# Reordering the work at the phase ends of an expert-choice mixture kernel

## The chip, the cores and the metric

The kernel runs on one core of one Trainium2 chip. The metric is the device time of one execution in microseconds (us), the median of the runs. Engines are named as in the profile: PE (TensorE matmuls), PEld (its weight loads), DVE (VectorE), ACT (ScalarE), POOL (GpSimd) and SP (SyncE, which only issues DMAs here).

## The reference

Three layers follow each other. An attention with gates and a running state gives 3072 token rows of 320 values. A mixture of 8 experts follows, each of which takes exactly 384 tokens: the pairs (token, expert) are taken in the order of their logit, and a pair is passed over if the token has an expert or the expert is full. The last layer multiplies two projections of each row and projects the product back.

```
logits = x @ w_gate                     # x: 3072 x 320, w_gate: 320 x 8
for idx in argsort(-logits.flatten()):  # greedy, capacity 384 per expert
    ... assigned[token] = expert
for e in range(8):
    h = maximum(x[mask_e] @ w1[e], 0)   # 320 x 1024
    out[mask_e] = h @ w2[e]             # 1024 x 320
a = out @ w_a; b = out @ w_b            # 320 x 1536 each
y = (a * b) @ w_out                     # 1536 x 320
```

## The kernel before

`attention` runs first (to about 200 us of the span) and is not touched. `experts` runs the rest as eight phases, one for each expert in the order in which the experts become full. A phase handles that expert's 384 tokens through both layers, and beside its matmuls the other engines find and fetch the tokens and weights of the next expert.

Every 32-bit operand is held as two parts, a high part (rounded to the matmul's type) and a low part (the rest). A product is summed from high by high, low by high and high by low. ACT writes high parts by a copy, DVE writes low parts by a subtraction that needs the high part first.

A phase k has two loops.

- Eight steps `f` (FT = 8): `up(k, f)` on PE, 8 matmuls into `psA[f % 2]`; ACT's relu writes `h_hi` (L1061); DVE's `h_low` writes `h_lo` (L1320); `down(k, f)` on PE, 9 matmuls into the three accumulators `acc`. PE issues `up(f + 1)` ahead of `down(f)`. `down(k, 0)` waits for `h_lo` and, accumulator by accumulator, for the three output copies of the phase before (`o_copied`, L895).
- Twelve steps `g` (GT = 12): `pair(k, g)` on PE, 16 matmuls into `psA` and `psB`; ACT copies `psA` to `a_sb` (L1080); DVE multiplies into `ab` (L1327); ACT writes `ab_hi` (L1075, `ab_high`); DVE writes `ab_lo` (L1331); `project(k, g)` on PE, 9 matmuls. The two DVE operations are one function, `product(g)`. In its step g, PE issues `pair(g + 1)` and then `project(g)`, DVE does `product(g + 1)`, and ACT does the `a_sb` copy and `ab_high(g)`.

The next expert's work is written into the twelve steps by hand. All engines take their instructions in the written order.

- Step 6: DVE's `rows` writes the row numbers `idx_g`. POOL then issues three gathers of 128 rows each into `xg` (L840), one semaphore each.
- The weights of the next expert come in four quarters q through two raw buffers, quarter q in buffer q % 2, four DMAs on SP each (L818 to L821). SP issues quarter q when the low parts of quarter q - 2 are done. ACT's `high_parts(k + 1, q)` (three copies, L1041 to L1043) waits for the four DMAs; DVE's `low_parts(k + 1, q)` (four subtractions, L1261 to L1268) waits for ACT. The table `SPLIT_AT` says after which step's product each quarter is split, on both engines: quarters 0 and 1 in steps 6 and 7, 2 in step 9, 3 in step 10.
- `widen(k + 1)` on DVE copies 64 columns inside each gathered tile (three copies, L1279), each after its gather has landed. It stands at the start of step 8.
- PE's `turn_tile(k + 1, t)` (L864) transposes gathered tile t into `psT`: tile 0 at the end of step 8, tiles 1 and 2 in steps 9 and 10 between `pair` and `project`. Tile t waits for widening copy t and for the low part of tile t - 1, since all three use `psT`. ACT's `columns(k + 1, t)` (L1033) copies the turned tile to `x1_hi`, DVE's `low(k + 1, t)` (L1284) writes `x1_lo`. DVE does `low(0)` at the start of step 9, `low(1)` and `low(2)` inside `product(10)` and `product(11)`, between its two operations.
- Step 11: PE waits for all of `x1`, issues `up(k + 1, 0)`, then `project(k, 11)`. At the end DVE copies the three accumulators to `o_sb` (L1408) and starts the next phase with `h_low(0)`.
- The search for the expert after next puts more small work on DVE: `leave_out` in step 7 after the product, `propose` in step 8 after it, `propose_rest` in step 9, `keys` in step 11.

The phases 0 to 5 are "search" phases, phase 6 ("rest") has no search, phase 7 prepares nothing. So there are seven phase ends at which a next phase is prepared.

Of the kernel before, what the change touches and what calls it, by code (L numbers as in the profile page):

```python
# [7 lines left out]
ALU = mybir.AluOpType  # L8
# [13 lines left out]
CAP = NT // E  # L22
# [639 lines left out]
ST = TILES // SC  # L662
SPLIT_EARLY = {0: 1, 2: 2, 4: 3}
WO_EARLY = 6
SPLIT_AT = {6: 0, 7: 1, 9: 2, 10: 3}
NG = 6
GJ = TILES // NG
GE = 72
# [2 lines left out]
def experts(nc, ctx, logit, identf, second, w_out, w1, w2, xs, out, fixed):  # L671
# [19 lines left out]
    FT = F1 // P  # L691
# [20 lines left out]
    h_hi = [sb(f"h_hi{n}", [P, CAP], F32R) for n in range(2)]  # L712
    h_lo = [sb(f"h_lo{n}", [P, CAP], F32R) for n in range(2)]
# [315 lines left out]
    @block.scalar  # L1029
    def _(act):  # L1030
        def columns(k, t, ps=psT):
            act.wait_ge(sm["t_done"], T * k + t + 1)
            act.copy(x1_hi[:, :, t * P:(t + 1) * P], ps[:, 0:3 * P].rearrange("p (j n) -> p j n", j=3)  # L1033
                     ).then_inc(sm["x1_hi_ready"], 1)

        def high_parts(k, q):
            n = q % 2
            act.wait_ge(raw_in[n], 64 * (2 * k + q // 2 + 1))
            if not (isinstance(k, int) and k == 0):
                act.wait_ge(sm["x2_mm"], 3 * k)  # L1040
            act.copy(w1_hi[q][:, :, :], w1_raw[n][:, :, :]).then_inc(sm["w_hi_done"], 1)  # L1041
            act.copy(w2_hi[q][:, :, 0:DM], w2_raw[n][:, :, :]).then_inc(sm["w_hi_done"], 1)
            act.copy(w2_hi[q][:, :, DM:], w2_raw[n][:, :, DM - 64:]).then_inc(sm["w_hi_done"], 1)  # L1043

        def high_out(q):
            act.wait_ge(wo_in[q % 2], 16 * (q // 2 + 1))
            act.copy(wo_hi[:, q * GQ:(q + 1) * GQ, :], wo_raw[q % 2]).then_inc(sm["wo_hi_done"], 1)

        high_parts(0, 0)
        for t in range(T):  # L1050
            columns(0, t, acc[t])

        def turn(k, beside):
            early = isinstance(k, int) and k == 0
            for f in range(FT):
                act.wait_ge(sm["up_done"], k * FT + f + 1)

                at_least(act, sm["down_done"], k * (FT - 1) + f - 1)
                if f == 0:
                    at_least(act, sm["x2_mm"], 3 * k)  # L1060
                act.activation(h_hi[f % 2][:, :], psA[f % 2][:, 0:CAP], ACT.Relu).then_inc(sm["h_hi_ready"], 1)  # L1061
                if early and f in SPLIT_EARLY:
                    high_parts(0, SPLIT_EARLY[f])
                if early and f == WO_EARLY:
                    high_out(0)
            for m in range(3):
                act.wait_ge(sm["x2_mm"], 3 * k + m + 1)
                act.copy(x2_hi[:, m, :], acc[m][:, 0:CAP]).then_inc(sm["x2_hi_ready"], 1)

            def ab_high(g):  # L1070
                act.wait_ge(sm["ab_done"], k * GT + g + 1)
                at_least(act, sm["out_done"], k * (GT - 1) + g - 1)
                if g < 2:
                    at_least(act, sm["out_mm"], T * k)
                act.copy(ab_hi[g % 2][:, :], ab[g % 2][:, :]).then_inc(sm["ab_hi_ready"], 1)  # L1075

            for g in range(GT):
                act.wait_ge(sm["ab_mm"], k * GT + g + 1)
                at_least(act, sm["ab_done"], k * GT + g - 1)
                act.copy(a_sb[g % 2][:, :], psA[g % 2][:, 0:CAP]).then_inc(sm["a_copied"], 1)  # L1080

                if beside and g > 9:
                    columns(k + 1, g - 9)
                ab_high(g)
                if early and g < Q - 1:
                    high_out(g + 1)
                if beside and g in SPLIT_AT:
                    high_parts(k + 1, SPLIT_AT[g])
                if beside and g == 9:
                    columns(k + 1, 0)  # L1090
        turns(act, turn)

    @block.vector
    def _(dve):
# [214 lines left out]
        per = ct.n - start + ROUNDS  # L1309
        start -= ROUNDS  # L1310

        def turn(k, beside):

            p = k + 1
            early = isinstance(k, int) and k == 0
            ct.turn(start + p * per)

            def h_low(f):
                dve.wait_ge(sm["h_hi_ready"], k * FT + f + 1)
                dve.scalar_tensor_tensor(out=h_lo[f % 2][:, :], in0=psA[f % 2][:, 0:CAP], scalar=0.0,  # L1320
                                         in1=f32(h_hi[f % 2][:, :]), op0=ALU.max, op1=ALU.subtract).then_inc(sm["h_ready"], 1)

            def product(g, turned=None):

                dve.wait_ge(sm["a_copied"], k * GT + g + 1)
                at_least(dve, sm["ab_ready"], k * GT + g - 1)
                dve.tensor_tensor(ab[g % 2][:, :], a_sb[g % 2][:, :], psB[g % 2][:, 0:CAP], ALU.mult).then_inc(sm["ab_done"], 1)  # L1327
                if turned is not None:
                    low(k + 1, turned)
                dve.wait_ge(sm["ab_hi_ready"], k * GT + g + 1)  # L1330
                dve.tensor_tensor(ab_lo[g % 2][:, :], ab[g % 2][:, :], f32(ab_hi[g % 2][:, :]), ALU.subtract  # L1331
                                  ).then_inc(sm["ab_ready"], 1)

            search = beside == "search"
            h_low(0)
            for f in range(FT - 1):
                if search and f:
                    narrow(p, f - 1)
                if search:
                    tally(p, f)  # L1340
                h_low(f + 1)
                if search:
                    is_full(p, f)
                if early and f in SPLIT_EARLY:
                    low_parts(0, SPLIT_EARLY[f])
                if early and f == WO_EARLY:
                    low_out(0)
            if search:
                narrow(p, FT - 2)
                tally(p, FT - 1)  # L1350
            for m in range(3):
                dve.wait_ge(sm["x2_hi_ready"], 3 * k + m + 1)
                dve.tensor_tensor(x2_lo[:, m, :], acc[m][:, 0:CAP], f32(x2_hi[:, m, :]), ALU.subtract).then_inc(sm["x2_ready"], 1)  # L1353
            if search:
                is_full(p, FT - 1)
                narrow(p, FT - 1)
            product(0)
            for g in range(GT):

                if search and FT + g < ROUNDS:  # L1360
                    tally(p, FT + g)
                    is_full(p, FT + g)
                if beside == "search" and g == 3:
                    give()
                if beside and g in (5, 6):
                    one_hot(p, 0 if g == 5 else SC - 1)
                if beside and g == 8:
                    widen(k + 1)
                if beside and g == 9:
                    low(k + 1, 0)  # L1370
                if g < GT - 1:
                    product(g + 1, g - 8 if beside and g in (9, 10) else None)

                if beside == "search":
                    if FT + g < ROUNDS:
                        narrow(p, FT + g)
                    if g == 3:
                        filled(p)
                    if g == 7:
                        leave_out()  # L1380
                    if g == 8:
                        propose()
                    if g == 9:
                        propose_rest()
                    if g == GT - 1:
                        keys()
                if beside == "rest" and g == 3:
                    the_rest(p)
                if beside and g == 4:
                    places(p)  # L1390
                if beside and g == 5:
                    one_hot(p, 1)
                    one_hot(p, 2)
                if beside and g == 6:
                    rows(p)
                if early and g < Q - 1:
                    low_out(g + 1)
                if beside and g in SPLIT_AT:
                    low_parts(k + 1, SPLIT_AT[g])
            if beside is None:  # L1400

                dve.wait_ge(sm["scattered"], 16 * T * (E - 1))
                dve.tensor_copy(idx_s[:, :], idx_g[:, :]).then_inc(sm["idx_s_ready"], 1)
            for t in range(T):
                dve.wait_ge(sm["out_mm"], T * k + t + 1)

                at_least(dve, sm["scattered"], 16 * T * k)
                dve.tensor_copy(o_sb[:, t, :], acc[t][:, 0:DM]).then_inc(sm["o_copied"], 1)  # L1408
# [39 lines left out]
```

## Time and profile before

| what | value |
|---|---|
| median of 3 runs | 985.36 us (981.37 to 985.89) |
| the profiled execution | 981.72 us |
| its span, first to last instruction | 980.0 us |
| mean granted PE clock | 0.949 of full |
| PE busy | 854.5 us (87%) |
| DVE busy | 650.0 us (66%) |
| ACT busy | 257.3 us (26%) |
| POOL busy | 187.9 us (19%) |

The profile is of one execution. Busy time is a sum of instruction durations; a matmul's end is modelled. In the rows of a timeline, instructions of one engine overlap a little, so that the distance between two starts says more of its pace than a duration does. The bracket at the end of a timeline row is the time that the engine was idle before the row, and who ended it. A "granted clock" of 1.00 is 2.4 GHz, 0.50 is 1.2 GHz.

### The profile page before, as it was taken

To read this page: it belongs to the slowest core of one execution; us is meant where nothing else is said; L and a number is where in the kernel's file an instruction comes from. 1 tells how busy PE (TensorE), PEld (TensorE's weight loads), DVE (VectorE), ACT (ScalarE), POOL (GpSimd) and SP (SyncE) were. 2 spreads that over 40 slices of the span, in tenths; PEclk is the share of its full clock that TensorE was granted. 3 is DMA by queue.
4 is the path that set the end of the run, shared out by engine and by line. 5 is a ranking of instruction groups with operands and counts; after the bars stand their busy time and mean duration, and the time that the engine had idled before them with its cause. 6 is when DMAs were issued, how large, how long until landed. Compare 5 with 4: busy or idle time off the path is not lost.

```text
span 980.0 us, 17872 instructions
## 1 busy us (share of the span) xinstructions
PE 854.5 (87%) x6122; PEld 809.0 (83%) x6122; DVE 650.0 (66%) x1639; ACT 257.3 (26%) x493; POOL 187.9 (19%) x218
## 2 busy tenths in 40 slices
PE   1899999943479979998999899899989998999995
PEld 1899899932378979997898799789978988998995
DVE  7489999975756775577558656855775575265222
ACT  5222222200223331232124123312331242233221
POOL 7466767710100110011001100110110011011001
PEclk9989999965689999999999999999999999999998
DMA  3866667200321220041013001200310040032000
GB/s 88 225 170 186 191 186 212 88 13 11 98 71 41 69 77 14 2 119 41 0 31 107 20 0 59 79 20 0 103 56 0 2 135 21 1 93 67 1 1 21
DMA packets 49722, 66.59 MB, mean 68 GB/s; under 512 B 6592, under 2 KB 43984, under 8 KB 48720
## 3 DMA queue, kind: packets, MB, share of 16 engines
q1 hardware_dynamic: 43856, 54.25, 19.4%
q0 software_dynamic: 2368, 7.88, 2.8%
q10 hardware_dynamic: 3456, 3.93, 1.2%
q8 instruction: 23, 0.38, 0.2%
q14 instruction: 19, 0.16, 0.1%
HBM read 57.88 MB, written 8.16 MB: 67 GB/s over the span
## 4 chain that ended last, share of the span: by engine, by line
PE 46%; DVE 20%; issue 5%; ACT 4%; DMA 1%; POOL 1%; DVEq 0%; ACTq 0%; POOLq 0%
PE psA L875 17%; PE acc L898 11%; PE psB L875 8%; PE acc L923 6%; DVE at_slot L1241 2%; DVE ab L1327 2%; DVE w_lo L1265 2%; ACT ab_hi L1075 2%; DVE w_lo L1261 2%; PE psT L935 2%; DMA xg<-xs_dram,idx_g 1%; DVE w_hi L1263 1%; DVE cmp L1103 1%; PE psT L949 1%; PE psT L943 1%
## 5 line engine op out<-in xcount | busy, mean ns | idle before, releaser
L875 PE MATMUL psA<-x_hi,wa 128*128 128x384 f32 x480 | 135.5, 347 | 0.4 <-DVE x_lo L1353 0.4
L875 PE MATMUL psB<-x_hi,wb 128*128 128x384 f32 x480 | 132.3, 341 | 0.0
L840 POOL DMA_INDIRECT xg<-xs_dram,idx_g x24 | 25.6, 1068 | 499.2 <-DVE idx_g L1255 494.3
L875 PE MATMUL psB<-x_lo,wb 128*128 128x384 f32 x288 | 97.0, 337 | 0.0
L875 PE MATMUL psA<-x_lo,wa 128*128 128x384 f32 x288 | 96.9, 336 | 0.0
L1080 ACT COPY a_sb<-psA 128x384 f32<-128x384 f32 x96 | 46.1, 480 | 188.8 <-PE psB L875 188.7
L923 PE MATMUL acc<-wo_hi,ab_hi 128*128 128x320 f32 x288 | 91.9, 319 | 1.0 <-DVE ab_lo L1331 1.0
L923 PE MATMUL acc<-wo_lo,ab_hi 128*128 128x320 f32 x288 | 88.8, 308 | 0.0
L923 PE MATMUL acc<-wo_hi,ab_lo 128*128 128x320 f32 x288 | 88.7, 308 | 0.0
L1331 DVE TENSOR_TENSOR ab_lo<-ab,ab_hi 128x384 fp32r<-128x384 f32 x96 | 53.5, 558 | 52.3 <-ACT ab_hi L1075 52.1
L1327 DVE TENSOR_TENSOR ab<-a_sb,psB 128x384 f32<-128x384 f32 x96 | 52.9, 551 | 52.4 <-ACT a_sb L1080 52.1
L875 PE MATMUL psA<-x_hi,w_hi 128*128 128x384 f32 x192 | 74.4, 388 | 14.1 <-DVE w_lo L1268 7.5
L875 PEld LDWEIGHTS psB<-x_hi,wb 128*128 128x128 f32 x480 | 86.2, 189 | 0.0
L875 PEld LDWEIGHTS psA<-x_hi,wa 128*128 128x128 f32 x480 | 83.0, 189 | 2.5 <-DVE x_lo L1353 1.1
L1061 ACT ACTIVATE h_hi<-psA 128x384 fp32r<-128x384 f32 x64 | 31.4, 491 | 202.7 <-PE psA L875 202.7
L898 PE MATMUL acc<-h_hi,w_hi 128*128 128x384 f32 x192 | 72.0, 375 | 14.3 <-DVE h_lo L1320 14.3
L1075 ACT CAST ab_hi<-ab 128x384 fp32r<-128x384 f32 x96 | 49.3, 514 | 88.3 <-DVE ab L1327 87.5
L875 PE MATMUL psA<-x_lo,w_hi 128*128 128x384 f32 x192 | 66.4, 346 | 0.0
L898 PE MATMUL acc<-h_hi,w_lo 128*128 128x384 f32 x192 | 66.3, 345 | 0.0
L898 PE MATMUL acc<-h_lo,w_hi 128*128 128x384 f32 x192 | 66.2, 345 | 0.0
L852 POOL DMA_INDIRECT out_dram<-o_sb,idx_s x24 | 23.6, 983 | 220.2 <-DVE o_sb L1408 215.4
L1320 DVE SCALAR_TENSOR_TENSOR h_lo<-psA,h_hi 128x384 fp32r<-128x384 f32 x64 | 34.9, 547 | 30.5 <-ACT h_hi L1061 30.5
(233 smaller groups left out, 1917.3 us busy)
## 6 DMA issues: line engine op xcount, KB each, us to landing
toks<-in_tok_dram SPq DMA_DIRECT2D x24, 484.0 KB, 5.1
w_raw<-in_w_dram SPq DMA_DIRECT2D x32, 320.0 KB, 3.2
w_raw<-in_w_dram SPq DMA_DIRECT2D x32, 256.0 KB, 3.0
qks<-in_qk_dram SPq DMA_DIRECT2D x24, 320.0 KB
w_raw<-in_w_dram SPq DMA_DIRECT2D x64, 64.0 KB, 2.8
xs_dram<-y ACTq DMA_DIRECT2D x24, 160.0 KB, 3.8
qst<-in_qk_dram SPq DMA_DIRECT2D x48, 60.0 KB
piece<-in_w_a_dram SPq DMA_DIRECT2D x6, 256.0 KB, 2.7
```

The lines of the kernel that those rows point to most:

```text
L840: pool.indirect_dma_start(out=xg[:, t, 0:DM], out_offset=None, in_=xrows, in_offset=bass.IndirectOffsetOnAxis(ap=idx_g[:, t:t + 1], axis=0 ...
L852: pool.indirect_dma_start(out=out, out_offset=bass.IndirectOffsetOnAxis(ap=idx_s[:, t:t + 1], axis=0), in_=o_sb[:, t, :], in_offset=None). ...
L875: last = pe.matmul(ps, w, x, start=(n == 0), stop=(n == len(steps) - 1))
L898: last = pe.matmul(acc[m][:, 0:CAP], w[q][:, f % FQ, c], x[n][:, :], start=(f == 0 and j == 0), stop=(f == FT - 1 and j == 2))
L923: last = pe.matmul(acc[t][:, 0:DM], x[n][:, c], w[:, g, :], start=(g == 0 and j == 0), stop=(g == GT - 1 and j == 2))
L935: last = pe.matmul(psG, ohc[:, n * GJ:n * GJ + GE // E, :].rearrange("p j e -> p (j e)"), cmp[:, js, :].rearrange("p j i -> p (j i)"), sta ...
L1061: act.activation(h_hi[f % 2][:, :], psA[f % 2][:, 0:CAP], ACT.Relu).then_inc(sm["h_hi_ready"], 1)
L1075: act.copy(ab_hi[g % 2][:, :], ab[g % 2][:, :]).then_inc(sm["ab_hi_ready"], 1)
L1080: act.copy(a_sb[g % 2][:, :], psA[g % 2][:, 0:CAP]).then_inc(sm["a_copied"], 1)
L1320: dve.scalar_tensor_tensor(out=h_lo[f % 2][:, :], in0=psA[f % 2][:, 0:CAP], scalar=0.0, in1=f32(h_hi[f % 2][:, :]), op0=ALU.max, op1=ALU.s ...
L1327: dve.tensor_tensor(ab[g % 2][:, :], a_sb[g % 2][:, :], psB[g % 2][:, 0:CAP], ALU.mult).then_inc(sm["ab_done"], 1)
L1331: dve.tensor_tensor(ab_lo[g % 2][:, :], ab[g % 2][:, :], f32(ab_hi[g % 2][:, :]), ALU.subtract).then_inc(sm["ab_ready"], 1)
```

## The change

Four edits, all in the order of instructions; no operation is added or left out.

1. Quarter 2 of the weights is split in step 8 instead of step 9, on ACT and on DVE (`SPLIT_AT`).
2. ACT's `columns(k + 1, 0)` moves from the end of step 9 to between its `a_sb` copy and `ab_high(9)`, as tiles 1 and 2 have it.
3. DVE's widening moves from the start of step 8 (before `product(9)`) to the end of step 7, before the low parts of quarter 1.
4. DVE's `h_low(k + 1, 0)` moves in front of the three output copies of phase k.

```
-SPLIT_AT = {6: 0, 7: 1, 9: 2, 10: 3}
+SPLIT_AT = {6: 0, 7: 1, 8: 2, 10: 3}
...
-                if beside and g > 9:
+                if beside and g >= 9:
                     columns(k + 1, g - 9)
                 ab_high(g)
...
                 if beside and g in SPLIT_AT:
                     high_parts(k + 1, SPLIT_AT[g])
-                if beside and g == 9:
-                    columns(k + 1, 0)
...
+        h_low(0, 0)
+
         def turn(k, beside):
...
-            h_low(0)
             for f in range(FT - 1):
...
-                h_low(f + 1)
+                h_low(k, f + 1)
...
-                if beside and g == 8:
-                    widen(k + 1)
                 if beside and g == 9:
                     low(k + 1, 0)
...
+                if beside and g == 7:
+                    widen(k + 1)
                 if beside and g in SPLIT_AT:
                     low_parts(k + 1, SPLIT_AT[g])
+            if beside is not None:
+                h_low(k + 1, 0)
             if beside is None:
```

## Rows read from the trace of the kernel before

**Rows 1.** Waits, whole run: us in total, times, longest us.
```profile
PE acc L898 <- DVE h_lo L1320: 14.3, 7, 2.4
PE psT L864 <- DVE xg L1279: 8.5, 6, 1.6
PE psA L875 <- DVE x_lo L1284: 6.6, 7, 1.2
PE psT L864 <- DVE x_lo L1284: 6.0, 7, 1.7
```

**Rows 2.** Timeline of PE, end of phase 2: start us, us, what.
```profile
530.22 0.55 PE L864 MATMUL psT<-identf,xg 128*128 128x128 f32 x3 [1.51 <-DVE xg L1279]
...
534.13 0.52 PE L864 MATMUL psT<-identf,xg 128*128 128x128 f32 x3 [0.53 <-DVE x_lo L1284]
...
535.80 0.52 PE L875 MATMUL psA<-x_hi,wa 128*128 128x384 f32 x2
...
541.34 0.44 PE L875 MATMUL psA<-x_hi,w_hi 128*128 128x384 f32 x1 [0.89 <-DVE x_lo L1284]
...
548.07 0.44 PE L898 MATMUL acc<-h_hi,w_hi 128*128 128x384 f32 x1 [2.38 <-DVE h_lo L1320]
```

**Rows 3.** Timeline of DVE, the same stretch, from the end of `leave_out`.
```profile
527.23 0.36 DVE L1208 TENSOR_TENSOR tiefree<-tie,free 128x192 f32<-128x192 f32 x1
527.74 0.69 DVE L1261 TENSOR_TENSOR w_lo<-w_raw,w_hi 128x512 fp32r<-128x512 f32 x1
...
529.98 0.39 DVE L1279 COPY xg<-xg 128x64 f32<-128x64 f32 x3
530.29 0.55 DVE L1327 TENSOR_TENSOR ab<-a_sb,psB 128x384 f32<-128x384 f32 x1
...
533.42 0.56 DVE L1284 TENSOR_TENSOR x_lo<-psT,x_hi 128x384 fp32r<-128x384 f32 x1 [0.33 <-ACT x_hi L1033]
...
540.27 0.55 DVE L1327 TENSOR_TENSOR ab<-a_sb,psB 128x384 f32<-128x384 f32 x1
...
544.18 0.17 DVE L1133 TENSOR_SCALAR sign<-best 128x24 int32<-128x24 int32 x1
...
546.18 1.28 DVE L1408 COPY o_sb<-acc 128x320 f32<-128x320 f32 x3
547.38 0.55 DVE L1320 SCALAR_TENSOR_TENSOR h_lo<-psA,h_hi 128x384 fp32r<-128x384 f32 x1
```

**Rows 4.** Timelines of POOL and SP, the same stretch: last gather, last load of quarter 2.
```profile
525.23 0.95 POOL L840 DMA_INDIRECT xg<-xs_dram,idx_g  x1 [0.30 <-issue]
...
526.43 0.44 SPq L821 DMA_DIRECT2D w_raw<-in_w_dram  x1
```

**Rows 5.** Line views: landing of that gather, of that load, of all 24 gathers.
```profile
DMA to landing us min/median/max: 4.3/4.3/4.3
...
DMA to landing us min/median/max: 4.0/4.0/4.0
...
DMA to landing us min/median/max: 3.1/3.7/5.0
```

**Rows 6.** Timeline of ACT, the same stretch.
```profile
531.36 0.83 ACT L1041 CAST w_hi<-w_raw 128x768 fp32r<-128x768 f32 x1
...
532.93 0.46 ACT L1033 CAST x_hi<-psT 128x384 fp32r<-128x384 f32 x1
...
538.83 0.48 ACT L1080 COPY a_sb<-psA 128x384 f32<-128x384 f32 x1 [1.70 <-PE psB L875]
```

**Rows 7.** Timeline of PE at the end of phase 6.
```profile
898.21 0.44 PE L898 MATMUL acc<-h_hi,w_hi 128*128 128x384 f32 x1 [0.21 <-DVE h_lo L1320]
```

**Rows 8.** Windows after phase 1's end: span, engines' busy us, granted clock, DMA, GB/s.
```profile
456.90:457.90 1.00, 1.00 (x10) 0.94 (x11) 0.03 (x1) 0.00 (x0) 0.70 (x2) 0.88 0.15 56
457.90:458.90 1.00, 1.00 (x4) 1.00 (x5) 0.91 (x3) 0.00 (x0) 0.69 (x2) 0.50 0.29 108
...
460.90:461.90 1.00, 1.00 (x7) 0.80 (x6) 0.54 (x3) 0.00 (x0) 0.00 (x0) 0.91 0.00 0
```

More of the change, by code:

```diff
@@ L664 @@
 WO_EARLY = 6
-SPLIT_AT = {6: 0, 7: 1, 9: 2, 10: 3}
+SPLIT_AT = {6: 0, 7: 1, 8: 2, 10: 3}
 NG = 6
@@ L1080, in turn @@
                 act.copy(a_sb[g % 2][:, :], psA[g % 2][:, 0:CAP]).then_inc(sm["a_copied"], 1)
-                if beside and g > 9:
+                if beside and g >= 9:
                     columns(k + 1, g - 9)
@@ L1088, in turn @@
                     high_parts(k + 1, SPLIT_AT[g])
-                if beside and g == 9:
-                    columns(k + 1, 0)
         turns(act, turn)
@@ L1310, in _, with h_low @@
         start -= ROUNDS
+        def h_low(k, f):
+            dve.wait_ge(sm["h_hi_ready"], k * FT + f + 1)
+            dve.scalar_tensor_tensor(out=h_lo[f % 2][:, :], in0=psA[f % 2][:, 0:CAP], scalar=0.0,
+                                     in1=f32(h_hi[f % 2][:, :]), op0=ALU.max, op1=ALU.subtract).then_inc(sm["h_ready"], 1)
+        h_low(0, 0)
         def turn(k, beside):
@@ L1316, in turn @@
             ct.turn(start + p * per)
[L1318 to L1321, printed above, removed]
             def product(g, turned=None):
@@ L1334, in turn @@
             search = beside == "search"
-            h_low(0)
             for f in range(FT - 1):
@@ L1340, in turn @@
                     tally(p, f)
-                h_low(f + 1)
+                h_low(k, f + 1)
                 if search:
@@ L1366, in turn @@
                     one_hot(p, 0 if g == 5 else SC - 1)
-                if beside and g == 8:
-                    widen(k + 1)
                 if beside and g == 9:
@@ L1397, in turn @@
                     low_out(g + 1)
+                if beside and g == 7:
+                    widen(k + 1)
                 if beside and g in SPLIT_AT:
                     low_parts(k + 1, SPLIT_AT[g])
+            if beside is not None:
+                h_low(k + 1, 0)
             if beside is None:
```

## The prediction
> **What bounds the kernel now.** I read the waits of the whole run first. At the seven phase ends TensorE loses time in four places, and these alone name what the change moves: for the next phase's first low part of h (14.3 us), for the widened tile (8.5), for the low part of the last turned tile in front of the next `up` (6.6), and for the low part of the tile before in front of a turning (6.0), together 35.4 us [rows 1]. Then the timelines of one phase end, phase 2's. On TensorE the reader sees the four stalls in their order: 1.51 us before tile 0 is turned, 0.53 before tile 1, 0.89 before `up(k+1, 0)` and 2.38 before `down(k+1, 0)`, 5.3 us in all [rows 2]. On VectorE he sees why: from 527.7 to 547.9 it works nearly without a gap, the longest one shown being 0.33 us [rows 3]. So inside a phase TensorE sets the time, but over the last 20 us of it VectorE does. An order that leaves VectorE more idle there makes the phase longer, whatever it does for TensorE's single waits. Last the transfers, since two edits move a wait for a DMA forward in an in-order queue.
>
> **The widening, one step earlier.** VectorE is done with `leave_out` at 527.6 [rows 3]. The third gather was issued at 525.23 and took 4.3 us, so it lands at 529.5 [rows 4, 5]. Today the widening comes at 529.98 and finds all three landed; in its new place VectorE stands still for 1.9 us with quarter 1's low parts and `product(9)` queued behind. After it the low parts of quarter 1 take 529.98 - 527.74 = 2.24 us: VectorE reaches `product(9)` at 529.7 + 2.2 = 531.9 instead of 530.29. What is gained is that tile 0 can be turned when TensorE comes to it, at 530.22 - 1.51 = 528.7.
>
> **Quarter 2, one step earlier.** ScalarE now comes to quarter 2's high parts before `a_sb(9)`. Quarter 2's last load was issued at 526.43 and took 4.0 us: 530.4 [rows 4, 5]. That issue hangs on the low parts of quarter 0, which stay where they were. ScalarE waits for it, copies for 532.93 - 531.36 = 1.57 us [rows 6] until 532.0, and only then does the `a_sb` copy (0.48): `product(9)` starts at 532.5, 0.6 us behind what VectorE's own queue gives. Cost of this wait alone: 0.6 us; it would be 2 us if the widening weren't late too. Product and `propose` take 533.42 - 0.33 - 530.29 = 2.80 us [rows 3], to 535.3. And now the step that decides: the low parts of quarter 2 (2.24 us) stand in front of `low(0)`, where they used to come behind `product(10)`. `low(0)` starts at 537.6 instead of 533.42. TensorE turns tile 1 0.71 us after that start [rows 2, 3], at 538.3 instead of 534.13, and since `project(9)` and `pair(11)` are queued behind the turning, all of it is 4.2 us late. Edit 2 (`columns(0)` in front of `ab_high(9)`) hides: tile 0 has been turned for 3 us, the copy is over before `ab(9)` is ready. At worst, uncovered, it costs its 0.48 us; at best it gives back the 0.33 us for which `low(0)` waited.
>
> **What is given back.** From tile 1's turning `pair(11)` follows after 1.67 us and `a_sb(11)` 3.03 us later [rows 2, 6]: 543.0, product at 543.5 instead of 540.27 [rows 3], 3.3 us late. VectorE itself is there earlier, at 537.6 + (540.27 - 533.42 - 2.24) = 542.2, so it is TensorE that has it wait. From `ab(11)` to `keys` 3.91 us, `keys` 2.00 us [rows 3]: 549.4. There edit 4 helps. Today three copies (1.20 us) stand before the low part of h and TensorE starts 0.69 us after its start, 1.89 us after `keys` [rows 2, 3]. Then the low part is first, the first copy follows 0.46 us later and lasts 0.48 with some 0.15 to be seen: 1.1 us. It gives 0.8 us (bounds 0, if the accumulators were late, and 1.2, all copies gone from the path). `down(k+1, 0)` starts at 550.5 instead of 548.07: **2.5 us later per phase end**. In TensorE's ledger: the stalls of 1.51 and 0.89 go, 2.38 becomes about 1.6, and 0.53 becomes 6.2 us (tile 0 turned at 528.7, the following pair done at 528.7 + 3.38 = 532.1, tile 1 at 538.3).
>
> For the six search phases I take 2.5 us each, 15.0. The gather's flight, which now counts, is up to 5.0 us in other places [rows 5], 0.7 more than in phase 2; I add 0.2 for each of the seven, 1.4 in all. Phase 6 has no search work, TensorE waits there only 0.21 us for the low part of h [rows 7], so edit 4 gives nearly nothing back; between 2.5 (as the others) and 4.2 (nothing given back) I take 3.3, since without `propose` the chain to `low(0)` is shorter. Sum 19.7 us. Nothing moves outside the phase ends: `h_low(0, 0)` of the first phase stays in place.
>
> **The clock.** After phase 1's end the granted clock falls to half and comes back within 5 us; the missing parts of the windows (0.12, three times 0.50, 0.09) sum to 1.7 us [rows 8]. The same follows in 4 of the 7 phase ends, all with a stall of 2.3 to 2.4 us before them; after the stalls of about 1.5 us at the widening it never does. The new stall is 6.2 us. I take it that each of the seven draws one slow stretch, and that it counts in full, since TensorE is what VectorE waits for behind tile 1's turning; and that the 1.6 us left at the end draw none. That is 7 x 1.7 - 4 x 1.7 = +5.1 us. Bounds: no stall draws any, -6.8; each draws twice as much, +17.
>
> The Trainium skill, TensorE: Matmul & The Clock Gate, What's actually happening, says it harder: "the default state is throttled, and activity releases the throttle". By it no long stall would be spared, and the sum is the one above, +24.8 us; by the share seen in the trace, 4 of 7, the clock's term would be 0 and the sum 19.7.
>
> **Sum.** 19.7 + 5.1 = 24.8 us on the profiled execution's 981.7: 1006.5. That execution lies 3.6 us under the median shown (985.36), with one run of three beside it and two above, a distance of about two slow stretches. If those hang on chance at 2.4 us and not at 6.2, the new time varies less and adds less to the median: I take 1008.
>
> **Rivals.**
> 1. The same chain, but the clock isn't drawn to half by the longer stall, or in few phases. For it: three stalls of 2.4 us were spared. Against: 6.2 us is two and a half times that. 981.7 + 19.7 - 6.8 = 994.6 without any slow stretch, 1001 with as many as now.
> 2. The slow stretches get longer or come twice per phase end, once behind each stall: 7 x 3.4 - 6.8 = +17, 1018.
> 3. The transfers land before ScalarE and VectorE come to them. Then `ab(9)` starts at 530.2, `low(0)` at 535.2, tile 1 is turned at 535.9, and of its 1.8 us all is given back by edit 4 and by VectorE's missing wait: no change in length, 982 to 987 with the clock. Against it: both flights are read from rows.
> 4. Faster: the three removed waits win. Point from which it decides: `low(0)` starts before 535.2, which asks for 2.4 us less in front of it than I count, the length of one quarter's low parts; for instance if they overlapped with VectorE's waits for the transfers. At `low(0)` one microsecond before that point each end gains up to 1 us, the stall at the end falls under 2 us and the 6.8 us of slow clock go: 981.7 - 7 - 6.8 = 968, 975 at the point itself.
>
> **Chances.** Forecast 0.62, rival 1 0.18, rival 2 0.08, rival 3 0.06, rival 4 0.06. Within 0.5% (5 us, what a measurement here can tell from no change) falls most of rival 3: faster 0.06, same 0.06, slower 0.88. Range 993 to 1020: rival 1 without any slow stretch at the low end, rival 2 with two microseconds for the higher runs at the other.
>
> **What would show it.** In the profile after, TensorE's wait for VectorE's low part of a turned tile (L864) should rise from 6.0 to some 43 us, its waits for the widening vanish but for those near zero, and the wait in front of `down` fall to about 11 us. VectorE should show a wait of about 1.9 us for the gather in each phase, ScalarE about 5 us per phase for the raw weights. Half clock should follow tile 1's turning in all seven phase ends. I am wrong if tile 1 is turned less than 2 us later than now against its phase, if ScalarE doesn't wait for the load, or if the phase ends' distance doesn't grow by 2.5 to 4.5 us.

## The result, and the profile after

The changed kernel takes 1012.33 us (median of 4, 1010.59 to 1016.36) against 984.5 us of the kernel before on the same chip: ratio 1.0307, 95% interval 1.0283 to 1.0332. 1008 was forecast. The profiled execution took 1013.25 us, its span is 1011.5 us, 31.5 more than before, with a mean granted clock of 0.929.

The waits of the whole run, as [rows 1] has them for before (engine and what it waited for: us in total, times, longest):

```profile
ACT w_hi L1041 <- DMA w_raw<-in_w_dram: 77.2, 8, 40.4
PE psT L864 <- DVE x_lo L1282: 46.5, 7, 7.2
DVE xg L1277 <- DMA xg<-xs_dram,idx_g: 17.0, 11, 2.2
PE acc L898 <- DVE o_sb L1409: 9.0, 6, 1.6
PE psA L875 <- DVE x_lo L1282: 1.2, 1, 1.2
```

Of the four waits of [rows 1] the one for the widening is gone, and of the one before `up` a single wait of 1.2 us is left of 6.6. The wait before `down` fell from 14.3 to 9.0 us and has another releaser, the first output copy. One grew from 6.0 to 46.5 us: TensorE in front of tile 1's turning. ScalarE waits 5.3 us per phase for the raw weights ((77.2 - 40.4) / 7; the 40.4 us are a single wait before the phases).

Now phase 2's end, TensorE first [rows 2], then VectorE [rows 3], POOL and SP [rows 4] and ScalarE [rows 6]. The third gather is issued at 532.19 here and at 525.23 before: take 6.96 off a time to lay it beside the prediction.

```profile
545.38 0.87 PE L864 MATMUL psT<-identf,xg 128*128 128x128 f32 x3 [6.71 <-DVE x_lo L1282]
...
548.45 0.84 PE L875 MATMUL psA<-x_hi,wa 128*128 128x384 f32 x2
...
554.03 0.45 PE L875 MATMUL psA<-x_hi,w_hi 128*128 128x384 f32 x1
...
559.89 0.45 PE L898 MATMUL acc<-h_hi,w_hi 128*128 128x384 f32 x1 [1.50 <-DVE o_sb L1409]
```

```profile
536.20 0.20 DVE L1277 COPY xg<-xg 128x64 f32<-128x64 f32 x1 [1.23 <-DMA xg<-xs_dram,idx_g]
536.33 0.69 DVE L1259 TENSOR_TENSOR w_lo<-w_raw,w_hi 128x512 fp32r<-128x512 f32 x1
...
539.48 0.55 DVE L1327 TENSOR_TENSOR ab<-a_sb,psB 128x384 f32<-128x384 f32 x1 [0.82 <-ACT a_sb L1080]
...
542.43 0.69 DVE L1259 TENSOR_TENSOR w_lo<-w_raw,w_hi 128x512 fp32r<-128x512 f32 x1
...
544.68 0.55 DVE L1282 TENSOR_TENSOR x_lo<-psT,x_hi 128x384 fp32r<-128x384 f32 x1
...
552.95 0.55 DVE L1327 TENSOR_TENSOR ab<-a_sb,psB 128x384 f32<-128x384 f32 x1 [3.48 <-ACT a_sb L1080]
...
556.88 0.17 DVE L1131 TENSOR_SCALAR sign<-best 128x24 int32<-128x24 int32 x1
...
558.89 0.55 DVE L1312 SCALAR_TENSOR_TENSOR h_lo<-psA,h_hi 128x384 fp32r<-128x384 f32 x1
559.35 1.27 DVE L1409 COPY o_sb<-acc 128x320 f32<-128x320 f32 x3
```

```profile
532.19 0.95 POOL L840 DMA_INDIRECT xg<-xs_dram,idx_g  x1 [0.30 <-issue]
```

```profile
533.40 0.44 SPq L821 DMA_DIRECT2D w_raw<-in_w_dram  x1
```

```profile
537.41 0.83 ACT L1041 CAST w_hi<-w_raw 128x768 fp32r<-128x768 f32 x1 [4.96 <-DMA w_raw<-in_w_dram]
...
538.98 0.47 ACT L1080 COPY a_sb<-psA 128x384 f32<-128x384 f32 x1
539.35 0.48 ACT L1033 CAST x_hi<-psT 128x384 fp32r<-128x384 f32 x1
```

| step, phase 2 | forecast | measured less 6.96 |
|---|---|---|
| `product(9)` starts | 532.5 | 532.52 |
| quarter 2's low parts start | 535.3 | 535.47 |
| `low(0)` starts | 537.6 | 537.72 |
| tile 1 is turned | 538.3 | 538.42 |
| `product(11)` starts | 543.5 | 545.99 |
| first low part of h | 549.4 | 551.93 |
| `down(k+1, 0)` starts | 550.5 | 552.93 |

Up to the turning the order gives what it was worked out to give, within 0.2 us. Then 2.4 us more are lost in one place, between the turning and `product(11)`, where VectorE waits 3.48 us for TensorE. TensorE's clock is at half for most of that time, and what is missing of it makes up these 2.4 us. The windows of that stretch (span, busy us of PE, PEld, DVE, ACT, POOL, granted clock, DMA share, GB/s), to be laid beside [rows 8]:

```profile
542.50:543.50 1.00, 0.00 (x0) 0.00 (x0) 0.97 (x2) 0.00 (x0) 0.00 (x0) 1.00 0.43 155
543.50:544.50 1.00, 0.00 (x0) 0.00 (x0) 0.93 (x3) 0.00 (x0) 0.00 (x0) 0.65 0.00 0
544.50:545.50 1.00, 0.12 (x1) 0.15 (x2) 1.00 (x3) 0.00 (x0) 0.00 (x0) 0.50 0.00 0
...
549.50:550.50 1.00, 1.00 (x5) 1.00 (x4) 0.00 (x0) 0.00 (x0) 0.00 (x0) 0.50 0.00 0
550.50:551.50 1.00, 1.00 (x7) 1.00 (x6) 0.00 (x0) 0.00 (x0) 0.00 (x0) 0.93 0.00 0
```

The granted clock falls to half (1.2 GHz) inside the stall and stays there until 550.6, 5.2 us after the turning; 2.6 us of clock are missing in these 5.2. In the kernel before, each of the four slow stretches at the phase ends began with TensorE's return or up to 1.5 us after it.

### The profile page after: what moved, and what is told of

Read it like the earlier page. It is cut to its first block, busy times and chain, and to the rows that moved or that the text cites. A ratio compares the mean times of both kernels' runs of the same rounds, so it can differ in the third digit from the quotient of the medians.

```text
span 1011.5 us, 17871 instructions
## 1 busy us (share of the span) xinstructions
PE 862.8 (85%) x6122; PEld 818.6 (81%) x6122; DVE 652.1 (64%) x1639; ACT 256.8 (25%) x493; POOL 189.1 (19%) x218
## 4 chain that ended last, share of the span: by engine, by line
PE 48%; DVE 16%; issue 5%; ACT 4%; DMA 3%; SPq 1%; POOL 1%; DVEq 0%; ACTq 0%
PE psA L875 18%; PE acc L898 10%; PE psB L875 9%; PE acc L923 7%; DMA w_raw<-in_w_dram 3%; DVE at_slot L1239 2%; DVE w_lo L1263 2%; DVE ab L1327 2%; ACT ab_hi L1075 2%; PE psT L935 2%; DVE w_lo L1259 2%; PE psT L949 1%; DVE cmp L1101 1%; DVE w_hi L1261 1%; ACT a_sb L1080 1%
## 5 line engine op out<-in xcount | busy, mean ns | idle before, releaser
L875 PE MATMUL psA<-x_hi,wa 128*128 128x384 f32 x480 | 139.8, 357 | 0.6 <-DVE x_lo L1352 0.6
L875 PE MATMUL psA<-x_lo,wa 128*128 128x384 f32 x288 | 99.6, 346 | 0.0
L923 PE MATMUL acc<-wo_hi,ab_hi 128*128 128x320 f32 x288 | 95.7, 332 | 1.0 <-DVE ab_lo L1331 1.0
L923 PE MATMUL acc<-wo_lo,ab_hi 128*128 128x320 f32 x288 | 92.1, 320 | 0.0
L923 PE MATMUL acc<-wo_hi,ab_lo 128*128 128x320 f32 x288 | 92.0, 319 | 0.0
L875 PEld LDWEIGHTS psA<-x_hi,wa 128*128 128x128 f32 x480 | 87.0, 197 | 2.2 <-issue 1.0
L923 PEld LDWEIGHTS acc<-wo_hi,ab_hi 128*128 128x128 f32 x288 | 57.1, 198 | 1.2 <-DVE ab_lo L1331 1.2
```

What stands on the lines that cost most here:

```text
L875: last = pe.matmul(ps, w, x, start=(n == 0), stop=(n == len(steps) - 1))
L923: last = pe.matmul(acc[t][:, 0:DM], x[n][:, c], w[:, g, :], start=(g == 0 and j == 0), stop=(g == GT - 1 and j == 2))
```

## The experiments

Each kernel was timed in five rounds beside the kernel before on its chip. Ratios are to that kernel, with their 95% intervals.

**Each edit alone.** The first kernel has only the new table:

```
-SPLIT_AT = {6: 0, 7: 1, 9: 2, 10: 3}
+SPLIT_AT = {6: 0, 7: 1, 8: 2, 10: 3}
```

> Only quarter 2's split moves from step 8+1 to step 8, on ScalarE and VectorE; the widening, columns(0) and the first low part of h stay as before. Theory (the forecast's chain): this edit alone makes the change slow. ScalarE's a_sb(9) stands behind the load of quarter 2 until 532.0 of phase 2, product(9) starts at 532.5 instead of 530.3, low(0) stands behind 2.24 us of low parts at 537.6, tile 1 is turned 4.2 us late with a stall of about 4.7 us before it (1.5 us stay before tile 0), down(k+1, 0) 3.3 us late. Seven times, 23 us, and with slow stretches behind every middle stall 5 to 12 us more: 1012 to 1020, slower than the full change or equal. Rival (the widening is the cost, the split is not): 984 to 990.

Measured: 1020.09 us against 982.0, ratio 1.0378 (1.034 to 1.0416), the upper end of what was expected. It is slower than the full change, and the wait is where it was forecast:

```profile
PE psT L864 <- DVE x_lo L1284: 36.4, 7, 5.4
```

That is 5.2 us per phase end, and 8.5 us in all are still lost for the widening in the same stretch (1.5 us in each of five ends). The rival falls: this edit alone is enough.

Only the widening moved:

```
-                if beside and g == 8:
-                    widen(k + 1)
...
+                if beside and g == 7:
+                    widen(k + 1)
                 if beside and g in SPLIT_AT:
```

> Only the widening moves in front of quarter 1's low parts. Theory: product(9) is 1.6 us late, in phases 0 and 6 2.2, since VectorE stands for the third gather with those low parts behind it; tile 0 is turned at once, TensorE's stall moves before tile 1 (about 3.3 to 3.6 us). VectorE bounds the end, so the phase end is 1.4 us late: 7 x 1.5 = 10 us, and up to 5 us for slow stretches behind the middle stall: 995 to 1000. Rival (the widening's edit is a gain since 1.5 us of stall go): 974 to 980.

Measured: 999.18 against 982.0, 1.0171 (1.014 to 1.0202). The wait for the widening has vanished from TensorE's waits, and the one before tile 1 has taken its place and more, the first row of the two below; the second is VectorE at phase 2's end, which stands for the third gather with quarter 1's low parts behind it.

```profile
PE psT L864 <- DVE x_lo L1284: 29.9, 7, 4.8
```

```profile
537.69 0.20 DVE L1279 COPY xg<-xg 128x64 f32<-128x64 f32 x1 [1.95 <-DMA xg<-xs_dram,idx_g]
```

Only the first low part of h moved:

```
+            if beside is not None:
+                h_low(k + 1, 0)
             if beside is None:
...
             for t in range(T):
                 dve.wait_ge(sm["out_mm"], T * k + t + 1)
```

> Only the first low part of h moves in front of the three output copies. Theory: 0.8 us less per phase end for six, 0.2 for the last: 5 us; the stall at the end falls from 2.4 to about 1.6 us and then draws no slow stretch, which gives back up to another 6.8 us: 973 to 980, likeliest 975. Rival (the copies bound down anyway): 984, no change.

Measured: 971.2 against 982.0, 0.9898 (0.9869 to 0.9926). The gain of 10.8 us is larger than the expected range allowed (973 to 980). The two terms of the theory are both there: the stalls before `down` fall from 14.3 to 9.0 us in the sum, and at the ends no slow stretch follows any more. Its stall before `down`, and the windows around it:

```profile
543.70 0.45 PE L898 MATMUL acc<-h_hi,w_hi 128*128 128x384 f32 x1 [1.49 <-DVE o_sb L1411]
```

```profile
540.00:544.00 4.00, 2.51 (x16) 2.19 (x15) 3.72 (x14) 0.69 (x2) 0.00 (x0) 1.00 0.00 0
544.00:548.00 4.00, 4.00 (x32) 3.72 (x31) 2.38 (x9) 0.31 (x1) 2.93 (x3) 1.00 0.22 82
```

Only `columns(k + 1, 0)` moved (`g > 9` to `g >= 9`, the copy at the end of step 9 gone):

> Only ScalarE's columns(0) moves between the a_sb copy and ab_high(9). Theory: it is covered; low(0) starts at most 0.1 us earlier, ab_high(9) 0.2 us later: 984, within 1.5 us of before. Rival (in front of ab_high it holds product(9) up, since tile 0 is turned late when the widening is late): up to 0.5 us per phase end, 988.

Measured: 977.91 against 982.0, 0.9958 (0.9937 to 0.9979). A small gain of 4 us where I expected none: of the phase ends' stalls only the one before tile 1 in phases 0 and 6 got shorter (6.0 to 3.8 us in the sum), and in this execution three slow stretches follow the phase ends instead of four. Together they make up the 4.2 us by which the phases of the profiled execution are shorter, 2.5 without the missing clock and 1.7 with it. How much of the median's 4 us is the clock is not shown; neither the theory nor the rival expected a gain.

**Without edit 1.** The other three together:

> The full change without edit 1 (quarter 2 split in step 9 on both engines): the widening before quarter 1's low parts, columns(0) in front of ab_high(9), the first low part of h in front of the copies. Theory: edit 3 alone gave 999.2; edit 4 takes 0.8 us per end and the slow stretches at the ends (5 and 3 us), edit 2 0.3 us per end: 988 to 992. TensorE's stall before tile 1 stays near 4 us, with half clock behind each. Rival (the widening costs only together with quarter 2's split): 970 to 975.

Measured: 989.53 against 980.81, 1.0085 (1.0052 to 1.0119). So edit 1 costs 2.2% on top of the others, and 3.8% alone: that fits the forecast, where the wait for the load costs 0.6 us behind a late widening and 2 us without it. The clock has a part in it that these two ratios don't separate.

**Which half of edit 1.** The full change, with VectorE's low parts of quarter 2 back in step 9:

```
+LOW_AT = {6: 0, 7: 1, 9: 2, 10: 3}
...
-                if beside and g in SPLIT_AT:
-                    low_parts(k + 1, SPLIT_AT[g])
+                if beside and g in LOW_AT:
+                    low_parts(k + 1, LOW_AT[g])
```

> The full change, except that VectorE does quarter 2's low parts in step 9 again, behind product(10); ScalarE does its high parts in step 8 as in the change. Theory: of the 4.2 us by which tile 1 is turned late, the 2.24 us of the split go and about 2 stay (the widening's wait and ScalarE's wait for the load, 0.6 beyond it). Stall before tile 1 about 4 us, phase end 1.0 us late, 7 us in all; a slow stretch behind each middle stall counts about 2 us (14), the slow stretches at the ends (7) and 5 us of edit 4 are gone with it: 990 to 1000, likeliest 996. Rival (ScalarE's early wait for the load is the main cost, not VectorE's order): 1008 to 1012, as the full change.

Measured: 993.21 against 980.7, 1.0128 (1.01 to 1.0155). ScalarE waits for the load as in the full change, and still 1.8% of the 3.1% are gone, the slow clock that goes with them included: the low parts in front of `low(0)` on VectorE are the larger part of what the change costs.

**The clock by itself.** The full change with matmuls in the stall whose result nobody uses:

```
+                if beside and g == 9:
+                    pe.wait_ge(sm["ab_done"], k * GT + g + 1)
+                    for _ in range(26):
+                        pe.matmul(psB[1][:, 0:CAP], wb[:, 0, 0:P], x2_hi[:, 0, :], start=True, stop=True)
                 if beside and 9 <= g < 8 + T:
                     turn_tile(k + 1, g - 8)
```

> The full change with 26 matmuls of 384 columns more per phase end, on TensorE in the long stall before tile 1 is turned (they start when ab(9) is there, use psB[1] which is free then, and their result is used by nobody). They do no work for the result. Theory: the stall of 5.1 to 7.2 us halves the clock behind it, 17.9 us in the trace of the change; with TensorE at work for some 4.5 us of the stall no slow stretch follows, and the kernel with 182 matmuls more is faster than the change: 993 to 998. Rival (the clock behind the stall costs nothing in the end, VectorE bounds there; or the fillers delay the turning): 1012 or more.

Measured: 998.83 against 980.7, 1.0184 (1.015 to 1.0217). It has 182 matmuls more than the full change and takes 12 us less by the two ratios (13.5 by the medians, 14.2 by the profiled spans). The fillers of phase 3, and the turning of tile 1 behind them, which still waits 0.52 us for VectorE:

```profile
630.22 4.78 PE L1012 MATMUL psB<-x_hi,wb 128*128 128x384 f32 x26 [1.77 <-DVE ab L1331]
635.52 0.52 PE L864 MATMUL psT<-identf,xg 128*128 128x128 f32 x3 [0.52 <-DVE x_lo L1286]
```

The 8 us from tile 1's turning on in phase 3, first of the full change, then of this kernel:

```profile
640.39:648.39 8.00, 8.00 (x35) 7.97 (x36) 3.03 (x9) 3.13 (x7) 0.00 (x0) 0.64 0.00 0
```

```profile
635.52:643.52 8.00, 8.00 (x50) 7.73 (x51) 5.46 (x13) 3.83 (x8) 0.00 (x0) 1.00 0.00 0
```

Thirty-five matmuls run in the one, 50 in the other, none of them a filler. In two of the seven ends a slow stretch came all the same, behind the 2.0 us of stall that is left in front of the fillers; with them it is just over the 993 to 998 expected. The five phases without one are 11.0 us shorter in the sum than those of the full change, which miss 13.0 us of clock behind their turnings: the slow clock there counts for more than four fifths of its length.

**A better order.** The widening in two parts (tiles 0 and 1 in step 7, tile 2 in step 8), with edits 2 and 4, quarter 2 in step 9:

```
                 if beside and g == 8:
-                    widen(k + 1)
+                    widen(k + 1, range(2, T))
...
+                if beside and g == 7:
+                    widen(k + 1, range(2))
                 if beside and g in SPLIT_AT:
```

> Edits 2 and 4 of the change; quarter 2 split in step 9 as before; of the widening, tiles 0 and 1 (landed by then) in front of quarter 1's low parts in step 7, tile 2 at its old place. Theory: VectorE bounds the phase end, so TensorE's stall of 1.5 us before tile 0 only moves before tile 1, as 1.7 us; VectorE saves the 0.33 us for which low(0) waited. Against edit 4 alone (971.2) 0.3 us per end, 2 us: 969; no slow stretches. Rival (the stall of 1.5 us before tile 0 counts in full): 971.2 - 8.5 = 962.

Measured: 969.06 against 980.7, 0.9879 (0.9848 to 0.9909). As expected, the wait for the widening has left TensorE's waits and one of 2.1 us stands before tile 1:

```profile
PE psT L864 <- DVE x_lo L1282: 12.7, 6, 2.1
```

Against edit 4 alone the phases got 0.35 us shorter, not 1.5.

On it, `h_low(k + 1, 0)` and the output copies in front of `keys()`, and the first `count` behind the third accumulator:

```
-                if between is not None and m == 0:
+                if between is not None and m == (2 if f == 0 else 0):
```

> As the kernel with two tiles widened early, but h_low(k+1, 0) and the three output copies stand in front of keys (2.0 us on VectorE) instead of behind it, and TensorE does the first count of down(k+1, 0) behind the third accumulator instead of the first. Theory: down(k+1, 0) finds its operands at once, the count then waits about 0.5 us for keys; 1.3 us per end for six ends: 8 us less than that kernel, 959 to 963. Rival (VectorE is the bound over the end as a whole, the keys are awaited in full by the count and the search behind it): within 2 us of that kernel, 967 to 970.

Measured: 972.17 against 980.7, 0.9924 (0.9898 to 0.9951). The theory falls, and the median lies above the rival's 967 to 970 too. The order gives nothing: its one search phase without a slow stretch is as long as those of the kernel it is built on, 88.66 and 88.65 us from one `down(k, 0)` to the next. The stall before `down` is gone, and the count and the search behind it wait for `keys`. The 3.1 us more go with the clock: it was 0.938 to 0.950 in these runs and 0.950 to 0.957 in those of the other kernel, whose profiled execution drew no slow stretch from the first phase end on, where this one drew six. Whether the order itself draws more of them is not shown.

Instead, VectorE's end made shorter: quarter 3's low parts in four pieces in the next phase, quarter 2's in step 10:

```
+LOW_AT = {6: 0, 7: 1, 10: 2}
...
+                if not early and 1 <= f <= 4:
+                    low_piece(k, 3, f - 1)
                 if search:
                     tally(p, f)
```

> The kernel with two tiles widened early (969.1), with VectorE's work at the end made shorter: quarter 3's four low part instructions go into the steps f = 1 to 4 of the next phase, one each, between narrow and tally, where VectorE waits 0.82 us for a count; quarter 2's low parts move from step 9 to step 10. Theory (VectorE bounds the phase end): 2.24 us less at the end, of which TensorE can use its stalls there, 0.9 + 1.5: 1.5 to 2.2 us per end, 954 to 959. Rival (TensorE's chain bounds it, as in the order keys last): 967 to 970.

Measured: 968.67 against 980.81, 0.9874 (0.9846 to 0.9902), no gain over the kernel it is built on. A miss: the theory had 954 to 959, the rival 967 to 970. Its phases without a slow stretch are 88.0 us, 0.7 shorter, but four stalls of 2.1 to 2.2 us before tile 1 drew slow clock in this execution. VectorE, relieved behind `low(0)`, now waits 1.42 us for TensorE before `ab(11)` in phase 2.

`low(0)` inside `product(9)`, where VectorE waits for `ab_hi` anyway:

```
-                if beside and g == 9:
-                    low(k + 1, 0)
                 if g < GT - 1:
-                    product(g + 1, g - 8 if beside and g in (9, 10) else None)
+                    product(g + 1, g - 8 if beside and g in (8, 9, 10) else None)
```

> The kernel with two tiles widened early (969.1), with low(0) between the two operations of product(9), as tiles 1 and 2 have it, instead of behind propose. Theory: the stall of 2.1 us before tile 1 goes; VectorE, which bounds the end, saves the 0.65 us for which ab_lo(9) waited: 0.5 us per end, 964 to 966. Rival (the stall before tile 1 counts in full): 954 to 957.

Measured: 964.6 against 980.81, 0.9828 (0.9803 to 0.9854), the theory's number: 88.1 to 88.3 us in phases 2 to 5. The stall before tile 1 goes, and 2.2 us come before `up`, where TensorE waits for a low part that stands behind quarter 2's on VectorE:

```profile
PE psA L875 <- DVE x_lo L1282: 14.5, 8, 2.2
```

Both moves in one kernel:

> Both of the two kernels before it in one: low(0) inside product(9), quarter 3's low parts in the next phase, quarter 2's in step 10. Theory: with VectorE relieved TensorE bounds the phase end; of its 4.5 us of stalls (2.1, 0.9, 1.5) about 3.5 go: 944 to 950. If VectorE is still the bound: 951 to 956.

Measured: 953.92 against 980.81, 0.9724 (0.9697 to 0.975), the fastest of all. Apart the two moves gave 4.5 and 0.4 us on the kernel with two tiles early, together 15. In a phase without a slow stretch, where the clock has no part, it is 0.5 and 0.7 us apart and 2.3 together. Waits of this kernel at the phase ends:

```profile
PE acc L899 <- DVE o_sb L1420: 9.0, 6, 1.6
PE psA L876 <- DVE x_lo L1291: 3.9, 8, 1.2
```

Of TensorE's 35.4 us [rows 1] 12.9 are left, nothing follows them at half clock, and phases 2 to 5 take 86.2 to 86.4 us. The 1.5 us before `down` stand still and the time is that of the weaker expectation, in which VectorE still bounds the last microseconds.

## Why the prediction was right, and where it was off

- **The bound.** Right. Over the last 20 us of a phase VectorE's order set the end, although "nearly without a gap" was read too kindly: between the rows shown VectorE also waits 0.65 us at 531.49 and 0.49 at 535.19, with the others 1.8 us in all. Removing single waits of TensorE (the two tiles early, the keys last) gave 0.35 us and nothing, while moving work away both before `low(0)` and behind it gave 2.3 us per phase. In the change itself TensorE, slowed, held the end up, as the forecast said of the time behind the turning.
- **The widening.** Right: VectorE stands 1.2 to 2.2 us for the third gather in its new place, with quarter 1's low parts behind it; alone it costs 1.7%, the clock included.
- **Quarter 2.** Right in its place and size: `low(0)` at the forecast time within 0.12 us. Putting VectorE's half back took 1.8 points of 3.1.
- **What is given back by edit 4.** Right: 0.8 us and a stall of 1.5 instead of 2.4. Alone it is a gain of 1.0%.
- **The chain without the clock.** From the first to the last `down(k, 0)` of the two traces the seven phase distances grew by 31.1 us. The missing clock behind tile 1's turning, summed over windows of 0.25 us, is 1.5, 2.0, 2.6, 2.9, 2.9, 2.9 and 3.0 us, 17.9 in all; before, it was four times 1.7 at the ends. If missing clock counts in full, 31.1 - 17.9 + 6.8 = 20.0 us, where 19.7 was forecast. It doesn't quite: by the kernel with fillers 11.0 of 13.0 us counted, and of the 1.7 us before, 1.4 (phases of 91.2 to 91.3 us with a slow stretch, 89.9 without). With these shares the chain is some 22 us (an estimate). So that 20.0 meets 19.7 this closely is in part luck.
- **The clock.** The term that was mis-sized. "Each of the seven draws one slow stretch" of 1.7 us gave 11.9; behind the turnings 17.9 us are missing. Less the 6.8 of before, that is 11.1 where 5.1 was forecast and rival 2 had 17. That all seven come and that the ends draw none was right. But a stretch of this stall lasts twice or three times as long as one of [rows 8] (3.4 to 5.1 us of clock missing) and begins in the stall: 29.0 us are missing in all, and 11.1 of them fall on idle time. Rival 2 had the longer stretches, and charged them in full. The kernel with fillers shows that TensorE's idleness in the stall brings them and that they count: 12 us back, with the same order of the rest. The 6.0 us too few here, some 4 by the shares above, are most of the difference between 24.8 and the 31.5 us by which the span grew.
- **Its own signs.** The waits came as listed: 46.5 us before a turning (some 43 forecast), 9.0 before `down` (11), 5.3 per phase for the raw weights (5). One sign failed in part: the phase distances were to grow by 2.5 to 4.5 us, and two of the seven grew by 5.4 and 5.7 (the others by 3.7 to 4.4, the mean is 4.4). These are phase 3, with 2.9 us of missing clock and no slow stretch before, and phase 6, with 3.0 and none.
- **A miscount.** "4 of the 7 phase ends" should have been 4 of 6: phase 6's end has a stall of 0.21 us. So two stalls of that length were spared, not three. It changes no term of the sum.
- **The median.** The forecast took 3.6 us for the distance of the profiled execution from the median and let 1.5 of them count; with the kernel before at 980.7 to 984.5 us in the later medians they were chance. The profiled execution was forecast at 1006.5 and took 1013.25; the 1.5 us added, and a median of 1012.33 below that execution, bring the two medians within 4.3 us. That part is luck.
- **The other rivals.** Rival 1 falls with half clock behind all seven turnings. Rivals 3 and 4 asked for `low(0)` at 535.2 and before; it started at 537.72, and both transfers landed after the engines had come to them.

## What to carry to other kernels

Before a step is moved earlier in an in-order queue, write down when its last operand lands, and who waits for the instructions behind it; here a wait of 1.2 to 2.2 us for a gather, moved forward to spare TensorE 1.5, made the kernel 1.7% slower. Where two engines take turns, relieve the one that is nearly without gaps, both of the work in front of the handover and of that behind it: here the move in front gave 4.5 us, the one behind 0.4, and the two together 15. A long stall of TensorE has to be counted with the slow clock behind it; here, matmuls of no use in stalls of 5 to 7 us made the kernel 1.2 points faster than idleness, and removing the stalls was better still.

## What the runs showed of the hardware

The counts are of the profiled executions, from the first phase end on; a slow stretch is counted to a stall when it began inside it or at most 1.6 us after it. Behind 51 stalls of 1.4 to 1.6 us before `down` (nine kernels) there was none, nor behind 22 of this length before a turning. Behind 49 stalls of 2.1 to 2.4 us (before `down` in four kernels, before tile 1 in four, before `up` in one) there were 24, from none of six to five of six in one execution. Of six stalls of 1.7 to 2.0 us in between, two were followed by one. Behind all 33 stalls of 3.6 to 7.2 us before tile 1 (five kernels), and behind one of 2.9, there was one. The length of the last stall isn't all of it: one stretch in the kernel with the keys last (at 635.0) began behind two waits of 0.8 and 0.6 us only. And the clock does not wait for TensorE's return: it fell in the middle of a 6.7 us stall.

The granted clock of a whole execution goes with its time. Of 17 executions of the kernel before on one chip the fastest (977.09 us) had 0.959 and the slowest (986.88) 0.945; where in those runs the clock was low is not recorded. In the profile, slow stretches hid the 0.7 us per phase of one experiment.

What a slow stretch costs depends on who is waited for. Behind a stall before `down` a phase with one was 1.4 to 1.7 us longer than one without. In the kernel with `low(0)` in `product(9)`, where the stretches came behind the stall before `up`, phases 3 to 5, each with one, took 88.1 to 88.3 us, and phase 2 without one 88.1. The stall of 1.5 us before `down` was gone in exactly these three: TensorE lost at half clock what it otherwise waited for VectorE.
